# One Trainium2 core, attention and two mixtures: a first-layer pass of 128 operand rows becomes one of 64, in alternating halves of the array

## The reference

```
h = np.maximum(x[mask] @ w1[e], 0.0)          # 192 -> 1024
out[mask] += top2_w[mask, k, None] * (h @ w2[e])   # first mixture, 1024 -> 192
...
h = np.maximum(x[mask] @ w1[e], 0.0)
out[mask] = gate_w[mask, None] * (h @ w2[e])       # second mixture
```

## Time and profile before

| | us |
|---|---|
| median of 3 runs (lowest, highest) | 1233.42 (1232.42, 1233.71) |
| the profiled execution, whole | 1230.78 |
| its span, first to last instruction | 1229.0 |
| TensorE matmuls busy | 1098.7 (89%) |
| TensorE weight loads busy | 1041.1 (85%) |
| VectorE, ScalarE, GpSimd busy | 753.6, 548.3, 523.5 |
| mean granted TensorE clock | 0.959 |

### The profile page before, as it was taken

One profiled execution on the slowest core, in us unless ns is written; L12 is line 12 of the kernel. 1 busy time (PEld: TensorE's weight loads), 2 busy tenths in 40 slices (PEclk: granted clock), 3 DMA queues, 4 the chain that ended last, 5 costly groups with the idle time before them and its releaser, 6 DMA issues.

```text
span 1229.0 us, 27241 instructions
## 1 busy us (share of the span) xinstructions
PE 1098.7 (89%) x8062; PEld 1041.1 (85%) x8062; DVE 753.6 (61%) x1412; ACT 548.3 (45%) x1543; POOL 523.5 (43%) x635
## 2 busy tenths in 40 slices
PE   1999168999999999999999999787289999999997
PEld 0566056999999999999999999766279999999997
DVE  8998896546465554646545464476854654466663
ACT  2112266445454544545445454356644554455552
POOL 5878102444444444444444444400324444444444
PEclk9999589999999999999999999989589999999999
DMA  9111200313122131312213111173712313124511
GB/s 330 67 58 65 60 1 21 95 42 95 38 73 67 41 102 42 94 38 79 64 41 97 39 37 38 40 257 104 239 50 72 100 39 102 40 61 128 141 56 36
DMA packets 51188, 97.89 MB, mean 80 GB/s; under 512 B 9651, under 2 KB 33051, under 8 KB 50876
## 3 DMA queue, kind: packets, MB, share of 16 engines
q1 hardware_dynamic: 33084, 61.77, 16.4%
q0 software_dynamic: 18048, 35.42, 9.9%
HBM read 69.62 MB, written 29.10 MB: 80 GB/s over the span
## 4 chain that ended last, share of the span: by engine, by line
PE 78%; DVE 13%; issue 3%; POOL 2%; ACT 2%; DMA 2%; DVEq 0%; POOLq 0%; ACTq 0%; SPq 0%
PE banks L605 22%; PE banks L607 11%; PE banks L591 9%; PE banks L597 7%; PE banks L596 7%; PE banks L592 7%; PE banks L593 7%; DVE prods L856 3%; PE banks L567 2%; POOL prods L415 2%; PE banks L575 2%; PE banks L576 2%; PE banks L529 1%; DVE choices L1064 1%; PE banks L519 1%
## 5 line engine op out<-in xcount | busy, mean ns | idle before, releaser
L1014 DVE SCALAR_TENSOR_TENSOR h_lo<-banks,h_hi 128x256 fp32r<-128x256 f32 x736 | 312.0, 424 | 373.6 <-ACT h_hi L743 319.0
L743 ACT ACTIVATE h_hi<-banks 128x256 fp32r<-128x256 f32 x736 | 282.5, 384 | 450.8 <-PE banks L597 340.1
L605 PE MATMUL banks<-w_hl,h_hi 128*128 128x384 f32 x1472 | 466.4, 353 | 0.0
L607 PE MATMUL banks<-w_hl,h_lo 128*128 128x192 f32 x1472 | 371.1, 252 | 0.0
L607 PEld LDWEIGHTS banks<-w_hl,h_lo 128*128 128x128 f32 x1472 | 279.6, 190 | 0.0
L605 PEld LDWEIGHTS banks<-w_hl,h_hi 128*128 128x128 f32 x1472 | 276.0, 188 | 0.2
L430 POOL DMA_INDIRECT x_slots<-token_rows,gather_idx x192 | 192.3, 1002 | 107.2 <-POOL gather_idx L427 76.8
L591 PE MATMUL banks<-x_hi_a,w_hi 128*128 (+1 forms) x736 | 224.9, 306 | 1.7 <-DVE x_hl_b L982 1.7
L592 PE MATMUL banks<-x_hi_a,w_lo 128*128 (+1 forms) x736 | 206.6, 281 | 0.0
L597 PE MATMUL banks<-x_hl_b,w_lo 128*128 (+1 forms) x736 | 206.3, 280 | 0.0
L596 PE MATMUL banks<-x_hl_b,w_hi 128*128 (+1 forms) x736 | 205.8, 280 | 0.0
(11 more groups left out here) (172 smaller groups left out, 1271.7 us busy)
## 6 DMA issues: line engine op xcount, KB each, us to landing
raw<-in_moe_w SPq DMA_DIRECT2D x17, 768.0 KB
choices<-choice_rows SPq DMA_DIRECT2D x28, 384.0 KB, 3.8
raw<-in_moe_w SPq DMA_DIRECT2D x17, 512.0 KB
raw<-in_moe_w SPq DMA_DIRECT2D x34, 256.0 KB
x_halo<-in_x SPq DMA_DIRECT2D x2, 2688.0 KB, 15.0
token_rows<-stage SPq DMA_DIRECT2D x14, 384.0 KB, 2.3
token_rows<-rows SPq DMA_DIRECT2D x14, 384.0 KB, 3.9
x_slots<-token_rows,gather_idx POOLq DMA_INDIRECT x192
```

The lines of the kernel that those rows point to most:

```text
L605: mm(y[:, i, 0:2 * D], h_hi[:, c % HBUFS, t], w2_hl[u][:, c, :, :], start=c == 0, stop=False)
L607: ins = mm(y[:, i, 0:D], h_lo[:, c % HBUFS, t], w2_hl[u][:, c, 0, :], start=False, stop=c == FC - 1)
L743: sc.activation(h_hi[:, c % HBUFS, :], banks[:, c % HBANKS, 0:BLOCK], ACT.Relu).then_inc(h_hi_ready[m], 1)
L1014: v.scalar_tensor_tensor(h_lo[:, c % HBUFS, :], banks[:, c % HBANKS, 0:BLOCK], 0.0, h_hi[:, c % HBUFS, :].bitcast(F32), ALU.max, ALU.subtr ...
```

## The change

The last of the five passes (L597 before) becomes a pass of 64 rows with the weights' low part and the tokens' high part alone; the product w_lo·x_lo of part b is left out, as it is for part a already.

- For chunks 0, 1, 2, 4 and 6 it uses partitions 0 to 63 and still ends the chunk.
- For chunks 3, 5 and 7 it uses partitions 64 to 127. It is issued right behind the one of the chunk before, begins its chunk's sum (`start=True`) in the next bank, and the other four passes of that chunk are added to it later. Before it stands a wait for `h_ready` of chunk c − 2 (c the even one), whose bank it starts to fill.
- A new tile `x_hi_b` holds the tokens' high part in partitions 64 to 127. ScalarE copies it there from `x_hl_b`, once a block at the end of the chunk loop (and once before the first block), and TensorE waits for it at c = 2 (`x_second`).

```diff
+FIRST_PAIR = 2
...
+        x_hi_b = sb("x_hi_b", [P, BLOCK], F32R)
...
+                def low_tail(x_parts, u, c, start):
+                    _, _, part_b = x_parts
+                    f = slice(c * P, (c + 1) * P)
+                    to = banks[:, c % HBANKS, 0:BLOCK]
+                    if not start:
+                        return mm(to, w1_lo[u][0:DB, 1, f], part_b[0:DB], start=False, stop=True)
+                    return mm(to, w1_lo[u][DB:P, 1, f], x_hi_b[DB:P], start=True, stop=False)
+
                 def first_product(x_parts, u, c):
...
-                    mm(to, w1_hi[u][:, 0, f], hi_a, start=True, stop=False)
+                    begun = c > FIRST_PAIR and c % 2 == 1
+                    mm(to, w1_hi[u][:, 0, f], hi_a, start=not begun, stop=False)
                     mm(to, w1_lo[u][:, 0, f], hi_a, start=False, stop=False)
                     mm(to, w1_hi[u][:, 0, f], lo_a, start=False, stop=False)
-                    mm(to, w1_hi[u][:, 1, f], part_b, start=False, stop=False)
-                    mm(to, w1_lo[u][:, 1, f], part_b, start=False, stop=True).then_inc(h_done[m], 1)
+                    ins = mm(to, w1_hi[u][:, 1, f], part_b, start=False, stop=begun)
+                    if not begun:
+                        ins = low_tail(x_parts, u, c, False)
+                    ins.then_inc(h_done[m], 1)
...
                         first_product(x_parts, u, c)
+                        if c >= FIRST_PAIR and c % 2 == 0:
+                            if c == FIRST_PAIR:
+                                pe.wait_ge(x_second[m], g + 1)
+                                pe.sem_inc(pe_tick, 1)
+                            pe.wait_ge(h_ready[m], g * FC + (c - 1 + LAG))
+                            low_tail(x_parts, u, c + 1, True)
...
+                def x_hi_second(g):
+                    _, _, part_b = x_buffers(parity(act, g))
+                    sc.copy(x_hi_b[DB:P], part_b[0:DB].bitcast(F32)).then_inc(x_second[m], 1)
...
+                act.wait_ge(x_hi_ready[m], 1)
+                x_hi_second(0)
...
+                        if c == FC - 1:
+                            act.wait_ge(x_hi_ready[m], g + 2)
+                            act.sem_inc(act_tick, 1)
+                            x_hi_second(g + 1)
```

More of the change, by code:

```diff
@@ L238, in attention_moe_moe @@
         x_split = [sem(f"x_split{m}") for m in range(2)]
+        act_tick = sem("act_tick")
+        x_second = [sem(f"x_second{m}") for m in range(2)]
         h_done = [sem(f"h_done{m}") for m in range(2)]
```

## The result

| | before | changed |
|---|---|---|
| median of the runs, us | 1233.08 (1232.42 to 1233.71, 4 runs) | 1371.08 (1370.55 to 1372.09, 4 runs) |
| ratio | | 1.1125 [1.1109, 1.1142] |
| profiled execution, whole | 1230.78 | 1371.19 |
| span | 1229.0 | 1369.5 |
| TensorE matmuls busy | 1098.7 | 1241.4 |

The kernel became 11% slower: 138 us, or 1.5 us for each of the 92 blocks. The forecast was slower, at 1260 us; the time lies 31 us above its range. The clock isn't in it.

The account below looks back on a forecast made before the run. TensorE was taken to bound the mixtures: 1230.8 + 59.8 for height changes − 33.1 for overlap = 1257.5 us, and with the runs' median 2.6 above the profiled execution, 1260. Range 1199 to 1340; the forecast's own, 1237 to 1320.

Parts of the forecast that it names:

- What bounds the kernel: In the two mixtures TensorE's matmuls fill 98% and all of the stretch, so a nanosecond there is one of the kernel.
- The overlap: First products: 64-row passes in opposite halves run at once, 276 pairs at 0.12 us, saving at most 33.1 us.
- My doubt about it: In a pair, two weight loads of 0.11 us must hide under one pass; if they can't, at most 5.5 us saved.
- Rival B: Pairs' loads go one after the other, no overlap, height changes free: 1233 us, or down to 1228; chance 0.18.
- The price of a change: Each switch between 128-row and 64-row passes on TensorE costs 0.065 us; 920 of them, 59.8 us.
- the upper end: Highest price allowed for one switch of pass height: 0.13 us, or 119.6 us for 920 switches.
- the one gap in the trace: L519 (128 rows) to L553 (8 rows): loads 0.24 us apart against 0.112, read as 0.13 for a row change.
- signs: Starts from L607 to the 64-row pass, and from the last one onward: 0.12 us if free, 0.18 forecast.
- ScalarE's copy and the new waits: Copy of about 0.37 us a block hidden in ScalarE's idle time, waits on `x_second` and `h_ready` free: nothing.
- Rival C: Full price for each height change on TensorE and no overlap of pairs; block period 11.1 us; chance 0.10.

Follow-up runs that it names:

- fourth_: Kernel before with a 64-row pass put fourth, tokens from a ScalarE copy awaited each block, computing 64 or all 128 output columns: 1565.17 and 1609.52 us.
- same_half: Changed kernel with both 64-row passes of each pair in partitions 0 to 63, so that they cannot overlap: 1402.18 us, ratio 1.1394.
- single64: Kernel before with only its fifth pass cut to 64 rows in all 8 chunks, no pairs, new waits or copy: 1509.52 us, ratio 1.226.
- single32: Kernel before with its fifth pass cut to 32 rows: 1512.00 us, ratio 1.2269.
- fourth_64x64: Kernel before with a 64-row pass put fourth, tokens from a ScalarE copy awaited each block, computing 64 of 128 output columns: 1565.17 us.
- single64_n128: Kernel before with its fifth pass cut to 64 rows and moving 128 of the 256 columns: 1471.13 us, ratio 1.1954.
- full_height: Changed kernel's order, waits and copy, but with all 128 rows in the passes that it had cut to 64: 1235.58 us, ratio 1.0031.

## Why the prediction was wrong

**What bounds the kernel** held: in the mixtures TensorE's time is the kernel's time. But for the wait in the two fourth_ runs, the changes in time are those in the spacing of TensorE's loads.

**The overlap** (33.1 us) held: 33 by same_half, with some 5 us of uncertainty, and equal starts in the trace. That the two numbers agree to the microsecond is luck. My doubt about it was misplaced. The load of 0.11 us is real and fills the spacing, but two loads into opposite halves start at the same instant (520.09 both). Rival B is refuted.

**The price of a change** is the step that failed. The text says "I take 0.065, half of the upper end". No run shows a price of 0.065. Measured (single64), it is 0.378 / 2 = 0.19, nearly three times that and beyond the upper end of 0.13. Both errors are in how I read the one gap in the trace. The gap was 0.24 between two loads, and I compared it with the spacing of 0.112 around it. But what lies between those loads is, by my estimate, a load (0.11), the streaming of 32 columns (0.34 / 384 × 32 = 0.03 by the earlier trace rows), and a rest: 0.24 − 0.11 − 0.03 = 0.10. With 256 columns at 0.11 in place of the 0.03, the same three terms give 0.32, which is what the changed kernel has. The spacing they replace is 0.12, so a change costs 0.20. The upper end was not an upper end, since it had been measured behind a pass much shorter than the ones it was used for. And halving it for the slower float32 passes was wrong: the 0.10 is the same behind L519 (full float32, one instance) and L607 (the faster format). The rest is 0.10 with 64 and with 32 rows (0.32 into a stay and 0.31 out of it in single64 and single32), with half the stationary columns (0.26 out of it in fourth_64x64, less an estimated 0.05 for half the load and 0.11 for the pass) and with half the moving ones (0.26 in single64_n128, less 0.11 and an estimated 0.05). At a change of columns alone it doesn't show: the 128\*64 turnings start 0.11 from their neighbours. What happens in the 0.10 no run shows. The distances between matmul starts that I had named as signs (0.18 on both sides by the forecast) came out as 0.21 and 0.32, and the rest of the second change shows one pass later: 0.28 from L618 to L620, where it was 0.18.

With 0.19 the sum would have been 1230.8 + 920 × 0.19 − 33.1 = 1372.5. Measured: 1371.2.

**ScalarE's copy and the new waits** were priced at nothing: full_height puts them at some 4 us together, with the reordering. TensorE has no row for `x_second` or `h_ready` among its waits in the changed kernel. The copy took 0.40 us against the 0.372 of its nearest row, and ScalarE was idle before the next ReLU all the same:

```profile
522.22 0.40 ACT L737 CAST x_hi_b<-x_hl_b 64x256 fp32r x1
523.17 0.38 ACT L769 ACTIVATE h_hi<-banks 128x256 fp32r<-128x256 f32 x1 [0.54 <-PE banks L596]
```

In fourth_64x64 nearly the same copy, needed two chunks earlier, cost 90 us. The cover was the time until it is needed, and not the copy's shortness.

**Rival C** came nearest, with the full price of 0.13 both ways and no overlap: 1233.4 + 119.6 = 1353. It was right that both changes pay in full; its size of the price was too small and the overlap wrong, and the two errors partly cancel in its 1353. I gave it 0.10.

None of the versions that I ran beats the kernel before. A stay costs 0.378 and a pair gives 0.12 back, so one stay would have to hold more than three pairs. A block has four in all, and the kernel has three banks for h. I haven't run such a version.

## What to carry to other kernels

Count the changes between passes of 128 rows and of 64 before counting what the halves save: here each cost 0.19 us, as much as one and a half passes of 256 columns, and the passes that gain must stand together in one stay. When a gap in a trace is to price something elsewhere, take it apart into load, streaming and rest before subtracting a spacing, and carry over only the rest. The pass over all rows can be the cheaper one even where half of them bring a product that nobody needs: with it (full_height) the same order took 1236 us and not 1371.

## What the runs showed of the hardware that I had not expected

- 64 and 32 rows cost the same (1509.5 and 1512.0 us); 96 cost as 128 (1236.4 us, with nothing at the pass). The step is somewhere between 96 and 64.
- Two passes of 64 rows in opposite halves start within 0.01 us of each other, with their weight loads (520.09).
- A load of 128 columns takes 0.11 us, by the distance to the next, with 128 rows and with 64, and in a steady stream it begins with the pass before it and is hidden, at full height (L597's load at 521.02, L596's pass at 521.01) and at half (same_half, L597's load at 524.32, 0.11 behind L596's). At a change between the two it isn't: it begins 0.32 or 0.31 us after the load before it, in place of 0.12.
